# Loading a first step's k and q unit by unit on two DMA queues in a fused gated-linear-attention and two-MLP kernel

## The reference

```python
f = 1.0 / (1.0 + np.exp(-f_logit))
state = np.zeros((B, H, D, D))
for t in range(S):
    state = f[:, :, t, :, None] * state + np.einsum('bhd,bhe->bhde', k[:, :, t], v[:, :, t])
    y[:, :, t] = np.einsum('bhd,bhde->bhe', q[:, :, t], state)
x = y.transpose(0, 2, 1, 3).reshape(B * S, H * D)
gate = 1.0 / (1.0 + np.exp(-(x @ w_gate)))          # 384 -> 1536
x = (gate * (x @ w_val)) @ w_out                    # 1536 -> 384
h = x @ w_in                                        # 384 -> 2048
out = (h * (1.0 / (1.0 + np.exp(-1.702 * h)))) @ w2_out
```

## Time and profile before

| | us |
|---|---|
| median of 3 runs | 933.9 (933.4 to 934.06) |
| the profiled execution | 933.81 |
| its span, first to last instruction | 932.1 |
| PE busy in the span | 920.3 (99%) |
| DVE, ACT, POOL busy | 434.8, 328.1, 137.6 |
| first matmul of the MLP starts at | 18.36 |

### The profile page before, as it was taken

How to read it: one execution, slowest core, us unless ns; L and a number is a source line. 1 busy time by engine, 2 the same in 40 slices (tenths; PEclk the granted TensorE clock), 3 DMA queues, 4 the chain that set the end, 5 groups by cost and what they waited for, 6 DMA issues and landing times.

```text
span 932.1 us, 17859 instructions
## 1 busy us (share of the span) xinstructions
PE 920.3 (99%) x7151; PEld 770.8 (83%) x7151; DVE 434.8 (47%) x793; ACT 328.1 (35%) x708; POOL 137.6 (15%) x181
## 2 busy tenths in 40 slices
PE   8999999999999999999999999999999999999997
PEld 6999988888888888888888888888888888888885
DVE  7987664465437445543422243443443443433433
ACT  3654433332334233332234432332332232333222
POOL 6323221122103211211024400000000000000000
PEclk9999999999999999999999999999999999999999
DMA  9843332213212321310143220110200100200001
GB/s 213 222 110 88 89 73 59 48 32 83 58 46 53 72 49 43 77 42 12 56 119 88 82 69 1 37 32 1 68 1 1 68 0 1 69 1 1 34 0 37
DMA packets 108182, 52.05 MB, mean 56 GB/s; under 512 B 95424, under 2 KB 100032, under 8 KB 108096
## 3 DMA queue, kind: packets, MB, share of 16 engines
q1 hardware_dynamic: 96432, 42.01, 18.0%
q10 hardware_dynamic: 11664, 8.85, 3.7%
HBM read 37.06 MB, written 9.44 MB: 50 GB/s over the span
## 4 chain that ended last, share of the span: by engine, by line
PE 96%; DVE 1%; issue 1%; POOL 1%; ACT 0%; ACTq 0%; POOLq 0%; DVEq 0%
PE all_ps L1261 31%; PE all_ps L1262 30%; PE all_ps L1263 30%; PE all_ps L1223 2%; PE all_ps L1245 1%; PE all_ps L1184 1%; PE all_ps L1254 1%; PE all_ps L1234 1%; PE all_ps L1300 0%; POOL k_dec L669 0%; DVE to_prod L957 0%; DVE x_lo L1016 0%; DVE after_prod L946 0%; ACT act_hi L855 0%; DVE w_lo L1032 0%
## 5 line engine op out<-in xcount | busy, mean ns | idle before, releaser
L1261 PE MATMUL all_ps<-x_hi,w_hi 128*128 128x512 f32 (+1 forms) x792 | 293.5, 371 | 0.7 <-DVE x_lo L1016 0.7
L1263 PE MATMUL all_ps<-x_hi,w_lo 128*128 128x512 f32 (+1 forms) x792 | 292.9, 370 | 0.0
L1262 PE MATMUL all_ps<-x_lo,w_hi 128*128 128x512 f32 (+1 forms) x792 | 292.8, 370 | 0.0
L1261 PE MATMUL all_ps<-act_hi,w_hi 128*128 128x512 f32 (+1 forms) x540 | 207.7, 385 | 0.8 <-DVE act_lo L1095 0.8
L1262 PE MATMUL all_ps<-act_lo,w_hi 128*128 128x512 f32 (+1 forms) x540 | 202.8, 375 | 0.0
L1263 PE MATMUL all_ps<-act_hi,w_lo 128*128 128x512 f32 (+1 forms) x540 | 202.4, 375 | 0.0
L855 ACT CAST act_hi<-act_f 128x512 fp32r<-128x512 f32 (+1 forms) x180 | 106.6, 592 | 233.5 <-DVE act_f L1081 161.1
L1261 PEld LDWEIGHTS all_ps<-x_hi,w_hi 128*128 128x128 f32 x792 | 149.2, 188 | 26.6 <-ACT act_f L849 0.6
L1263 PEld LDWEIGHTS all_ps<-x_hi,w_lo 128*128 128x128 f32 x792 | 149.2, 188 | 25.3
L1262 PEld LDWEIGHTS all_ps<-x_lo,w_hi 128*128 128x128 f32 x792 | 149.2, 188 | 25.1
L1095 DVE TENSOR_TENSOR act_lo<-act_f,act_hi 128x512 fp32r<-128x512 f32 (+1 forms) x180 | 119.0, 661 | 78.3 <-ACT act_hi L855 78.3
(11 more groups left out here) (97 smaller groups left out, 529.4 us busy)
## 6 DMA issues: line engine op xcount, KB each, us to landing
stage<-w SPq DMA_DIRECT2D x16, 384.0 KB, 3.3
x_dram<-final SPq DMA_DIRECT2D x36, 128.0 KB, 2.8
x_raw<-x_dram SPq DMA_DIRECT2D x6, 768.0 KB, 4.7
out_t<-final SPq DMA_DIRECT2D x18, 256.0 KB, 2.3
f_raw<-f_t SPq DMA_DIRECT2D x90, 48.0 KB, 2.2
k_raw<-k_t SPq DMA_DIRECT2D x88, 48.0 KB, 2.1
q_raw<-q_t SPq DMA_DIRECT2D x88, 48.0 KB, 2.1
stage<-w ACTq DMA_DIRECT2D x6, 576.0 KB, 4.3
```

The lines of the kernel that those rows point to most:

```text
L1261: pe.matmul(dst, w_hi[:, at:at + P], m_hi, start=first, stop=False)
L1262: pe.matmul(dst, w_hi[:, at:at + P], m_lo, start=False, stop=False)
L1263: return pe.matmul(dst, w_lo[:, at:at + P], m_hi, start=False, stop=last)
```

## The change

Five edits go together.

- **f.** Unit 1's f has a load of its own, issued by ACT as its first work, into the second f slot (DVE clears that slot, and POOL half of the tile that holds all four units' f). SP still loads f of all four units after f of unit 0; units 2 and 3 are read from it.
- **k and q.** SP loads k of the first step unit by unit: eight DMAs of 48 KB in the place of two of 192 KB. q of units 0 and 1 is issued by ACT, behind its second sigmoid, and q of units 2 and 3 by SP behind k: eight DMAs of 48 KB in all. Each unit has semaphores of its own.
- **POOL and DVE.** POOL takes k and q of unit 0 first, then clears `to_x`, and goes on with units 1, 2 and 3. It now makes q of units 0, 1 and 2, and DVE q of unit 3 alone, behind the first mask.
- **PE.** Each unit is turned and scored before the next is turned.
- **DVE behind that.** The remainders of x and of weight piece 0 are interleaved in another way, and the sum of y in block 3 stands ahead of the remainder of the weights.

In the diff the names are those of the lines above; `unit_of(t, n)` is the slice of one unit.

```diff
-                for i in range(PAIR):
-                    sp.dma_start(all_units(k_first[rows[i], :]), k_units[i, :, :, 0:C]).then_inc(first_k_loaded, 16)
+                for n in range(UG):
+                    for i in range(PAIR):
+                        sp.dma_start(by_batch(unit_of(k_first, n)[rows[i], :]), k_steps[n, i, :, :, 0:C]).then_inc(first_k_loaded[n], 16)
                 sp.wait_ge(q_gaps_set, 1)
-                for i in range(PAIR):
-                    sp.dma_start(all_units(q_first[rows[i], :]), q_units[i, :, :, 0:C]).then_inc(first_q_loaded, 16)
+                for n in range(2, UG):
+                    for i in range(PAIR):
+                        sp.dma_start(by_batch(unit_of(q_first, n)[rows[i], :]), q_steps[n, i, :, :, 0:C]).then_inc(first_q_loaded[n], 16)
...
 @block.gpsimd
-                for n in range(UG):
-                    decay_k(n)
+                decay_k(0)
+                decay_q(0)
+
+                pool.wait_ge(gate_done, UG)
+                pool.memset(to_x, 0.0).then_inc(rows_set, 1)
+                decay_k(1)
                 decay_q(1)
-                decay_q(3)
+                decay_k(2)
+                decay_k(3)
+                decay_q(2)
...
 @block.scalar
+                act.wait_ge(gaps_set, 2)
+                for i in range(PAIR):
+                    act.dma_start(by_batch(f_raw[rows[i], 1, :]), f_steps[1, i, :, :, 0:C]).then_inc(f_loaded[1], 16)
 
                 act.wait_ge(warm_set, 1)
                 act.activation(k_rows[:, 0, 0, 0:1], x_raw[:, 0, 0:1], ACT.Sigmoid)
                 forget(0)
                 forget(1)
+                act.wait_ge(q_gaps_set, 1)
+                for n in range(2):
+                    for i in range(PAIR):
+                        act.dma_start(by_batch(unit_of(q_first, n)[rows[i], :]), q_steps[n, i, :, :, 0:C]).then_inc(first_q_loaded[n], 16)
                 forget(2)
                 forget(3)
+                take_k(0)
...
 @block.vector
-                decay_q(0)
-                decay_q(2)
-                for n in range(UG):
+                after_visit(score_visit[0])
+                decay_last_q(UG - 1)
+                for n in range(1, UG):
                     after_visit(score_visit[n])
                 first_w1_second_part(0)
+                x_second_part(0, [0, 1])
                 first_w1_second_part(1)
-                x_second_part(0, [0])
+                x_second_part(0, [2])
                 first_w1_second_part(2)
-                x_second_part(0, [1, 2])
...
+                    if b.q == 3:
+
+                        add_y(VISITS[v][3], v)
                     if 0 < b.q < J1 and b.j + 2 < J1:
                         w1_second_part(b.j + 2)
...
 @block.tensor
+                for n in range(UG - 1):
+                    turn(n)
+                    visit(score_visit[n])
+                turn(UG - 1)
+                visit(score_visit[UG - 1])
                 for n in range(UG):
-                    turn(n)
-                for v in range(BEFORE_MLP):
-                    visit(v)
+                    visit(out_visit[n])
```

More of the change, by code:

```diff
@@ L150, in gla_moe_moe2 @@
         gaps_set = sem("gaps_set")
+        f_gaps_set = sem("f_gaps_set")
         q_gaps_set = sem("q_gaps_set")
@@ L157, in gla_moe_moe2 @@
         v_loaded = sems("v_loaded", 4)
-        first_f_loaded, first_k_loaded, first_q_loaded, first_v_loaded = (
-            sem(n) for n in ("first_f_loaded", "first_k_loaded", "first_q_loaded", "first_v_loaded"))
+        first_f_loaded, first_v_loaded = (sem(n) for n in ("first_f_loaded", "first_v_loaded"))
+        first_k_loaded, first_q_loaded = (sems(n, UG) for n in ("first_k_loaded", "first_q_loaded"))
         gate_done = sem("gate_done")
@@ L283, in wait_q_dec @@
         def wait_q_dec(eng, n):
-            if n in (0, 2):
-                eng.wait_ge(q_dec_by_dve, n // 2 + 1)
+            if n == UG - 1:
+                eng.wait_ge(last_q_dec_done, 1)
             else:
-                eng.wait_ge(q_dec_done, n // 2 + 1 if n < UG else n - 1)
+                eng.wait_ge(q_dec_done, n + 1 if n < UG else n)
         def wait_state(eng, n):
@@ L410, in gla_moe_moe2, with unit_of @@
         q_first = final_flat[:, 0:UG * W]
+        def unit_of(t, n):
+            return t[:, n * W:(n + 1) * W]
         Z_ZERO = PAIR * D
@@ L422, in gla_moe_moe2 @@
         f_steps, k_steps, q_steps = (t.rearrange("(b p) i d s -> p i d b s", b=B) for t in (f_t, k_t, q_t))
-        f_units, k_units, q_units = (t.rearrange("u i d s -> i d u s") for t in (f_t, k_t, q_t))
+        f_units = f_t.rearrange("u i d s -> i d u s")
         v_sides = v_n.rearrange("(c r p) t k e -> p r t c k e", r=SIDES, p=UG)
@@ L621, in _ @@
             def _(pool):
-                pool.memset(x_raw[:, 0, :], 0.0).then_inc(warm_set, 1)
+                pool.memset(f_first[:, 0:UG * W // 2], 30.0).then_inc(f_gaps_set, 1)
+                pool.memset(x_raw[:, 0, 0:384], 0.0).then_inc(warm_set, 1)
                 pool.memset(starts[:, :, :], SAFE_PRODUCT).then_inc(starts_set, 1)
@@ L647, in decay_q @@
                     if n < UG:
-                        pool.wait_ge(first_q_loaded, 32)
+                        pool.wait_ge(first_q_loaded[n], 32)
                     else:
@@ L704, in _ @@
                     take_end(n)
+                pool.wait_ge(scan_done, UG)
                 pool.wait_ge(p_end_done, UG)
@@ L750, in forget @@
                     u = Unit(n)
-                    if 0 < n < UG:
+                    if 1 < n < UG:
                         act.wait_ge(first_f_loaded, 32)
@@ L755, in forget @@
                     if n == 0:
-                        act.wait_ge(gaps_set, 8)
+                        act.wait_ge(gaps_set, 9)
                     if n == 2:
@@ L928, in _ @@
                 dve.memset(f_raw[:, 0, :], 30.0).then_inc(gaps_set, 1)
-                dve.memset(f_first, 30.0).then_inc(gaps_set, 1)
+                dve.memset(f_raw[:, 1, :], 30.0).then_inc(gaps_set, 1)
+                dve.memset(f_first[:, UG * W // 2:UG * W], 30.0).then_inc(gaps_set, 1)
                 dve.memset(k_first, 0.0).then_inc(gaps_set, 1)
@@ L1108, in _ @@
                         w1_second_part(b.j + 2)
-                    if v is not None and VISITS[v][3] is not None:
+                    if v is not None and VISITS[v][3] is not None and b.q != 3:
                         add_y(VISITS[v][3], v)
```

33 lines of the change are left out of this document (15 added, 18 removed).

## The result

The changed kernel takes 936.34 us (median, 935.6 to 937.66), the kernel before beside it 933.4: ratio 1.0029, interval 1.0021 to 1.0038. I predicted no change, 934.1 with a range of 932.4 to 935.6. The profiled execution took 936.24, its span is 934.3, and the granted clock over it 0.995 (0.999 before).

The account below looks back on a forecast made before the run. PE was taken to bound the kernel (96% of the chain), its ramp waits released by DVE from block 0's product on. Terms -0.15 + 0.55 - 0.13 = +0.3 us on 933.81 made 934.1, range 932.4 to 935.6.

Parts of the forecast that it names:

- P: Start of block 0's product on DVE (line 1101): 21.68 in the kernel before, forecast at 22.1.
- k of unit 0 at 7.8: First step, loads: unit 0's k lands at 7.8 us, bounds 7.5 and 9.35; POOL waited until 9.38 before.
- POOL's 5.0 us behind it, to 12.8: First step: POOL's seven products and a memset take 5.0 us from 7.8, so the last q product ends at 12.8.
- the sharing of which I had made a rival: Rival, first step's loads: q of units 0 and 1 shares with unit 0's k, landing at 9.0 or later; 935.3, chance 0.17.
- The serial chain of 2.9 behind the last product: First step, PE and ACT: from POOL's last product to placing y takes 2.9 us (2.1 before), so 15.7 against 15.86.
- 5.82 + 0.55 to block 0's product: From placing y to block 0's product on DVE: 5.82 us as before, plus 0.55 for a moved weights' remainder.
- Weights late (5 in 100): Rival: SP's later issues bring weight piece 1 after DVE wants it, a slip of 2.5 costing 1.3; 935.4, chance 0.05.
- The remainder of 0.55 bare ahead of the scan: DVE ahead of block 0: the remainder of weight piece 0's third part, formerly in a wait for x, costs +0.55 us.
- The sum of y -0.13: Block 3 on DVE: the sum of y ends at 37.66 rather than 37.79, since it waits for ACT's copies; -0.13 us.
- The signs I had said would show me wrong: Trace signs against the forecast: line 1101 on DVE starting before 21.5, or POOL's first product past 8.7.

Follow-up runs that it names:

- run 10: The kernel of run 5 with v of the first step issued by ACT, behind its four sigmoids, rather than by SP; 933.68 us, ratio 1.0001 to the kernel before.
- run 11: The kernel of run 10 with DVE's old order of the remainders of x and of weight piece 0; 933.54 us, ratio 1.0000 to the kernel before.
- Run 13: The kernel of run 11 with unit 3's turn ahead of unit 2's score on PE; 933.14 us, ratio 0.9996 to the kernel before.
- run 5: The changed kernel with seven dummy matmuls, which add nothing to the result, in PE's gaps of the first step; 934.44 us, ratio 1.0010 to the kernel before.
- run 8: The kernel before with six of PE's dummy matmuls in the wait for the first k left out; 935.26 us, ratio 1.0017 to the kernel before.
- run 6: The kernel of run 5 with DVE's old order of the remainders; 934.56 us, ratio 1.0008 to the kernel before.
- run 4: The changed kernel with DVE's old order of the remainders of weight piece 0 and x; 936.37 us, ratio 1.0027 to the kernel before.
- run 12: The kernel of run 11 without the seven dummy matmuls in PE's gaps; 934.54 us, ratio 1.0014 to the kernel before.
- Run 9: The kernel before with only the sum of y put ahead of the weights' remainder on DVE in block 3; 933.85 us, ratio 0.9999.

## Why the prediction was wrong

The forecast was P = 15.7 + 5.82 + 0.55 = 22.1. It came at 25.20. No rival named the clock: those whose numbers lie nearest (935.3, 935.4) rest on k landing late or DVE waiting for weights, and neither happened in the changed kernel. Step by step:

- **k of unit 0 at 7.8: right.** 7.86.
- **POOL's 5.0 us behind it, to 12.8: 0.7 short.** The last q product ended at 12.85 + 0.68 = 13.53. I had watched k against q of units 0 and 1, and let k win; I didn't ask when q itself lands. POOL's second product waited 0.56 for it, and two k products took 1.57 for 1.32, with DVE's q product starting beside them at 11.28 (I had allowed 0.15 for that). That q of unit 0, on ACT's queue, came 1.3 us after k may be the sharing of which I had made a rival, only with the loser changed; no run separates it from q's later issue. The rule that I weighed there, from the Trainium skill ("DMA: Bandwidth & Descriptors", section "Issuing engines are not separate DMA queues"), says that spreading saves issue time alone, which is usually small. The first half agrees with the trace. The second doesn't here: issue time was the limit, at 0.48 us for each DMA of 48 KB, with a DMA share of 0.29 to 0.60 from 10 to 13 us, and in run 10 block 0's product came 0.9 us earlier by it.
- **The serial chain of 2.9 behind the last product: 4.3 (13.53 to 17.85).** Its parts were right, as run 11 shows at full clock: last product at 12.52 + 0.88 = 13.40, placing at 16.43, 3.0. Run 13 took 0.54 of it away (12.98 to 15.47 is 2.5), where I had the chain 0.8 longer than in the kernel before (2.9 for 2.1). What I had missed is the clock.
- **5.82 + 0.55 to block 0's product: 7.35.** The clock again: the placing is 1.17 longer.
- **The clock is the failed step: it has no term in the sum.** I used PE's durations of the kernel before throughout and took them for properties of the operations. They held only while the clock did. The kernel before was as sparse from 10 to 13 us, but full from 13 on; the change leaves PE sparse for a microsecond more, and the clock fell at 13.4. 1.4 + 1.0 = 2.4 of the 3.1 us between forecast and result lie in stretches that the clock lengthened, the other 0.7 is mostly q's landing. The runs put the clock's price somewhat lower, since not all of it is on the path: keeping it (run 5) brings P forward by 1.80 and the median by 1.9, losing it alone (run 8) costs about 1.75 at P and 1.7 in the median. That is most of the 2.9 us; the rest is q, late weights and DVE's order, which no run parts cleanly.
- **Weights late (5 in 100): it was there.** Piece 1 was cast at 20.06 (18.46 before), and I had reckoned that a slip costs from 0.8 to 1.2 on. In the changed kernel the lost clock hid it; without that it is worth 0.9 at P (run 5 against run 10), and not as the wait of DVE that I had reckoned, but since POOL's cast then lies beside DVE's scan, 1.65 us for 0.69. In run 6 it is a wait, of 0.76.
- **The remainder of 0.55 bare ahead of the scan: there as a row, and a cost of 0.4 only once nothing else binds.** It stands at 22.66, without idle time, directly ahead of the scan, as predicted. The three pairs of runs with and without it (changed kernel and run 4, 5 and 6, 10 and 11) give ratios that differ by 0.0002 at most, which their intervals don't resolve. From the placing of y to P it is worth 0.39 with early weights (runs 10 and 11) and nothing with late ones (7.13 and 7.18 in runs 5 and 6). I had reckoned it whole.
- **The sum of y -0.13: right as far as the row goes.** PE's wait went from 0.56 to 0.48, too little for any median to show; a remainder of weights ahead of it was not the wait, ACT's copies were, as the row of DVE shows with the sum starting right behind them:

```profile
40.81 0.42 DVE L1020 TENSOR_TENSOR y_t<-y_t,all_ps 128x256 f32<-128x256 f32 x1 [1.09 <-ACT y_t L802]
```

The signs I had said would show me wrong, line 1101 or POOL's first product out of place, did half of their work: POOL's first product was where I wanted it, while line 1326, expected at 15.4 to 16.2, stood at 17.85, and line 1101, expected at 21.8 to 22.6, at 25.20. But the sentence on when I would be wrong named only a line 1101 that is too early; that it could be late by 3 us I hadn't thought of.

## What to carry to other kernels

Ahead of a change that cuts a wait of PE into several small ones, ask what the granted clock will do: take the PE durations behind it at both levels, and keep both ends for the range. When a load is cut into more DMAs, count the issues of everything behind it on that queue (here 0.48 us each), and if the queue runs empty of bytes, give some of them to another engine; the byte count alone says nothing. And when a product needs two inputs, forecast the landing of both.

## What the runs showed of the hardware

**The clock falls behind a sparse stretch, and comes back late.** PE was busy 0.73, 0.67 and 0.44 us of each us from 10 to 13 in the changed kernel, and the grant fell to 0.50 at 13.4. In run 8 it fell at 11.2, behind an idle time of 1.33 us in front of 10.77. It stayed low for 6.7 us in the changed kernel and 6.8 in run 8, for 3.4 in runs 4 and 12, although PE was busy for 5.5 of the 6 us from 14 to 20 in the first. The Trainium skill tells of a related pattern ("TensorE: Matmul & The Clock Gate", section "HAM oscillation — how this bites in real kernels"): where a burst of matmuls is shorter than the wait for a DMA behind it, PE comes out of the wait at the lower clock. Run 8's trace agrees, with bursts of 0.71 and 0.44 us and waits of 1.61 and 1.33 in front of them. The changed kernel's does so only for its last wait, 0.94 us behind a burst of 0.44; the three ahead of it, 0.27 to 0.32, are shorter than the bursts. And the kernel before, with bursts of 0.41 to 0.44 and waits of 0.55, is against it: it was as sparse from 10 to 13 and kept 1.00; only in the next us do the two part, 0.97 busy against 0.33. Windows of the kernel before:

```profile
11.00:12.00 1.00, 0.41 (x2) 0.20 (x2) 0.93 (x4) 0.37 (x1) 1.00 (x3) 1.00 1.28 239
12.00:13.00 1.00, 0.41 (x2) 0.20 (x3) 1.00 (x3) 0.37 (x1) 1.00 (x2) 1.00 1.12 254
13.00:14.00 1.00, 0.97 (x40) 0.83 (x43) 0.84 (x2) 0.37 (x1) 0.70 (x2) 1.00 1.06 349
```
Run 4 was as sparse as the changed kernel from 10 to 14 (0.64, 0.62, 0.44, 0.42) and kept the clock until 15. Which part of the stretch decides, no run here tells; seven dummies spread over it (run 5) kept the clock.

**Which of DVE and POOL gives way is decided by very little.** Two executions at the same place, the product of unit 4's q on POOL beside a weights' remainder on DVE. Run 9 first, POOL and DVE:

```profile
24.99 1.92 POOL L655 TENSOR_TENSOR q_dec<-q_raw,to_prod 128x256 f32<-128x256 f32 x1 [1.04 <-issue]
```

```profile
25.03 1.35 DVE L1032 TENSOR_TENSOR w_lo<-stage,w_hi 128x1152 fp32r<-128x1152 f32 x1
```

Run 10, POOL and DVE:

```profile
25.39 0.68 POOL L655 TENSOR_TENSOR q_dec<-q_raw,to_prod 128x256 f32<-128x256 f32 x1 [1.03 <-issue]
```

```profile
25.42 1.85 DVE L1052 TENSOR_TENSOR w_lo<-stage,w_hi 128x1152 fp32r<-128x1152 f32 x1
```

POOL starts first in both, by 0.04 and 0.03 us, and yet loses in one. The one that loses takes most of the other's time on top: 1.92 for 0.68, or 1.85 for 1.35. In run 9 POOL lost, and PE waited 1.59 us for it, where it waits 0.42 in the earlier trace rows. That single execution is therefore no witness on the sum of y.
